# Attention scores as zero-padded single products between the matmuls of an MLP, instead of pairs on two halves of the TensorE array

## The reference

```python
# r, k, v: (B=4, H=8, S=768, D=48); w, u: (H, D)
for t in range(S):
    cur = einsum('bhd,bhe->bhde', u * k[t], v[t])
    y[t] = einsum('bhd,bhde->bhe', r[t], state + cur)
    state = w[..., None] * state + einsum('bhd,bhe->bhde', k[t], v[t])
x = y.transpose(0, 2, 1, 3).reshape(3072, 384)
h = x @ w_in;  x = (h * sigmoid(1.702 * h)) @ w_out      # d_ff = 2048
h = x @ w_in2; x = (h * tanh(softplus(h))) @ w_out2
```

## Time and profile before

| | us |
|---|---|
| median of 3 runs | 945.72 |
| lowest and highest | 943.12 and 946.43 |
| the profiled execution, its own time | 943.12 |
| its span in the trace | 941.0 |

### The profile page before, as it was taken

How to read it: one execution, slowest core, us unless ns; L and a number is a source line. 1 busy time by engine, 2 the same in 40 slices (tenths; PEclk the granted TensorE clock), 3 DMA queues, 4 the chain that set the end, 5 groups by cost and what they waited for, 6 DMA issues and landing times.

```text
span 941.0 us, 11881 instructions
## 1 busy us (share of the span) xinstructions
PE 929.4 (99%) x4716; PEld 777.1 (83%) x4716; DVE 397.7 (42%) x683; ACT 171.1 (18%) x314; POOL 183.0 (19%) x157
## 2 busy tenths in 40 slices
PE   8989999999999999999999999999999999999998
PEld 7878888888888888888888888888888888888886
DVE  8375663443454343444335543233233333233322
ACT  0322311111111111111123331111111111111111
POOL 6665743331323231333000000000000000000000
PEclk8599999999999999999999999999999999999999
DMA  9652111220212021111043000000000000000000
GB/s 213 156 177 68 43 34 51 55 51 22 59 50 52 26 67 44 34 51 42 1 151 92 27 1 1 1 34 0 1 34 1 34 1 1 33 1 1 34 1 33
DMA packets 41029, 41.85 MB, mean 44 GB/s; under 512 B 27280, under 2 KB 33552, under 8 KB 40976
## 3 DMA queue, kind: packets, MB, share of 16 engines
q1 hardware_dynamic: 40976, 41.10, 15.7%
HBM read 36.37 MB, written 4.72 MB: 44 GB/s over the span
## 4 chain that ended last, share of the span: by engine, by line
PE 98%; DMA 1%; issue 0%; SPq 0%; DVE 0%; ACT 0%
PE h L767 44%; PE acc L786 42%; PE y_bank L695 4%; PE a_bank L679 2%; PE y_bank L704 2%; PE z_bank L719 2%; PE z_bank L732 1%; DMA arena<-in_rk 1%; PE h L719 1%; PE acc L679 0%; PE y_bank L679 0%; DVE arena L510 0%; SPq L219 0%; DVE arena L487 0%; ACT arena L449 0%
## 5 line engine op out<-in xcount | busy, mean ns | idle before, releaser
L591 DVE CAST g_hi<-act 128x512 fp32r<-128x512 f32 x192 | 91.6, 477 | 410.9 <-PE acc L786 392.1
L427 ACT ACTIVATE act<-h 128x512 f32<-128x512 f32 x192 | 114.7, 597 | 547.8 <-PE h L767 547.8
L767 PE MATMUL h<-x_hi,win_hi 128*128 128x512 f32 x576 | 186.7, 407 | 0.7 <-ACT x_hi L413 0.7
L767 PE MATMUL h<-x_hi,win_lo 128*128 128x512 f32 x576 | 184.3, 409 | 0.0
L767 PE MATMUL h<-x_lo,win_hi 128*128 128x512 f32 x576 | 183.9, 409 | 0.0
L786 PE MATMUL acc<-g_hi,wout_hi 128*128 128x512 f32 x576 | 172.5, 399 | 0.0
L786 PE MATMUL acc<-g_hi,wout_lo 128*128 128x512 f32 x576 | 166.3, 390 | 0.0
L786 PE MATMUL acc<-g_lo,wout_hi 128*128 128x512 f32 x576 | 165.9, 389 | 0.0
L593 DVE TENSOR_TENSOR g_lo<-act,g_hi 128x512 fp32r<-128x512 f32 x192 | 146.9, 765 | 6.6
L786 PEld LDWEIGHTS acc<-g_hi,wout_hi 128*128 128x128 f32 x576 | 108.3, 188 | 23.7
L786 PEld LDWEIGHTS acc<-g_lo,wout_hi 128*128 128x128 f32 x576 | 108.1, 188 | 23.0
(11 more groups left out here) (102 smaller groups left out, 593.0 us busy)
## 6 DMA issues: line engine op xcount, KB each, us to landing
arena<-in_rk SPq DMA_DIRECT2D x44, 192.0 KB, 3.3
mid<-in_wts SPq DMA_DIRECT2D x16, 384.0 KB, 6.8
arena<-in_wts SPq DMA_DIRECT2D x16, 384.0 KB, 3.3
arena<-in_k SPq DMA_DIRECT2D x22, 192.0 KB, 3.2
arena<-in_v SPq DMA_DIRECT2D x22, 192.0 KB, 3.2
arena<-in_r SPq DMA_DIRECT2D x21, 192.0 KB, 2.9
out<-mid SPq DMA_DIRECT2D x5, 768.0 KB, 3.3
mid<-in_rk SPq DMA_DIRECT2D x4, 192.0 KB, 7.6
```

The source lines that it names most:

```text
L427: act.activation(act1[:, f % 2], h_bank[f % 2][:, :], GATES[layer]).then_inc(g_done, 1)
L591: dve.tensor_copy(g_hi[:, f % 2], act1[:, f % 2]).then_inc(ghi_done, 1)
L767: ins = pe.matmul(hb, w[:, f, kd, :], x[:, par, kd, :], start=i + kd == 0, stop=i == 2 and kd == KD - 1)
```

## The change

`kz` is a new buffer with the decayed k of both halves, each 112 partitions high: `kz[:, 0]` holds the even heads in partitions 0 to 47 and zeros elsewhere, `kz[:, 1]` the odd heads in 64 to 111 and zeros elsewhere. GpSimd clears it once and then, for each chunk, writes the two 48-partition parts, and scales r in a third operation. The score product of a half is then 112 rows deep, with the zeros taking out the other head. It stands alone after one MLP matmul, like the other pieces.

Both halves go through `a_bank` and one `amat` buffer, one after the other: half 0 in phase 0 (j = 0 to 3), half 1 in phase 1 (j = 4 to 7). `inside` of half 0 comes in phase 1 at j = 0 to 3, that of half 1 in phase 2 at j = 0 to 3, and `before` moves to j = 4 to 7 of phase 2. `y_bank` holds no scores any more, so the wait for `x_done` moves from `scores` to `inside`. `prepare` of a chunk waits until the scores of the chunk before have been computed (`a_done`), since there is one `kz`.

In the opening the products stay 48 rows deep and in their old banks, but all four of half 0 come first and then all four of half 1. The dummy matmuls become 20 of 128x128 in place of 8 of these and 24 smaller ones.

```diff
-WARM = 8
+WARM = 20
...
+        kz = part(2 * HP * CH)[0:PR_ROWS, :].rearrange("p (a h t) -> p a h t", a=2, h=HP)
...
-        amat = [part(HP * CH).rearrange("p (h t) -> p h t", h=HP) for _ in range(2)]
+        amat = part(HP * CH).rearrange("p (h t) -> p h t", h=HP)
...
+            pool.memset(kz, 0.0).then_inc(cleared, 1)
...
                 pool.wait_ge(rk_in[b], a * 32 + 32)
-                pool.tensor_tensor(e.rk, e.rk, decay, ALU.mult).then_inc(r_dec, 1)
+                pool.wait_ge(a_done, n * 2)
+                for j, p0 in enumerate((0, ODD)):
+                    if j:
+                        pool.wait_ge(kz_done, n * 2 - 2 * B + 1)
+                    pool.tensor_tensor(kz[p0:p0 + D, j], e.rk[p0:p0 + D, 1], decay[p0:p0 + D, 1], ALU.mult).then_inc(kz_done, 1)
+                pool.wait_ge(kz_done, n * 2 - 2 * B + 2)
+                pool.tensor_tensor(e.rk[:, 0], e.rk[:, 0], decay[:, 0], ALU.mult).then_inc(r_dec, 1)
...
-                if phase == 0 and b < B:
-                    for half in range(2):
-                        select(n, later[b], later_scores[half], half)
+                if phase < 2 and b < B:
+                    select(n, later[b], a_bank, phase)
...
+                else:
+                    if hp == 0:
+                        pe.wait_ge(kz_done, n * 2 - 2 * B + 2)
+                        pe.wait_ge(r_dec, n + 1)
+                        pe.wait_ge(sel_done, n * 2 + half)
+                    ins = pe.matmul(a_bank[:, hp * CH:(hp + 1) * CH], kz[:, half, hp, :], later[b].rk[:, 0, hp, :], start=True, stop=True)
...
-                    if phase == 0 and j == 0:
-                        scores(n, b)
-                    if phase == 1 and j // 4 < 2:
-                        inside(n, b, j // 4, i, a)
+                    if phase == 0 and j // 4 == 0:
+                        scores(n, b, 0, i)
+                    if phase == 1 and j // 4 == 0:
+                        inside(n, b, 0, i, a)
+                    if phase == 1 and j // 4 == 1:
+                        scores(n, b, 1, i)
                     if phase == 2 and j // 4 == 0:
+                        inside(n, b, 1, i, a)
+                    if phase == 2 and j // 4 == 1:
                         before(n, b, i)
```

More of the change, by code:

```diff
@@ L101, in operands @@
         def operands(b):
-            return Buffers(rk=rk[b % 2], ks=ks[b % 2], vs=vs[b % 2], rr=rr, amat=amat)
+            return Buffers(rk=rk[b % 2], ks=ks[b % 2], vs=vs[b % 2], rr=rr, amat=[amat, amat])
         STG0 = FIRST
@@ L147, in mlp_rwkv_program @@
         first_scores = [[a_bank, h_bank[0]], [acc[0], acc[1]]]
-        later_scores = [a_bank, y_bank]
         first_update = h_bank[1]
@@ L165, in mlp_rwkv_program @@
         dtab = sem("dtab")
+        kz_done = sem("kz_done")
         r_dec = sem("r_dec")
@@ L385, in chunk @@
                         split(f)
-            pool.wait_ge(cleared, 4)
+            pool.wait_ge(cleared, 5)
             pool.wait_ge(ds_done, B)
@@ L511, in _ @@
                 if b == 0:
-                    dve.tensor_tensor(amat[0][0:PR_ROWS], decay[:, 1], wide(powers[:, LOGS - 1, 0, :], CH), ALU.mult).then_inc(dsrc, 1)
+                    dve.tensor_tensor(amat[0:PR_ROWS], decay[:, 1], wide(powers[:, LOGS - 1, 0, :], CH), ALU.mult).then_inc(dsrc, 1)
             def split(win, wout):
@@ L665, in decay_rows, with scores @@
                 for hp in range(HP):
-                    ins = pe.transpose(z_bank[:, hp * PR_ROWS:(hp + 1) * PR_ROWS], amat[0][0:PR_ROWS, hp, :], ident[0:PR_ROWS, 0:PR_ROWS])
+                    ins = pe.transpose(z_bank[:, hp * PR_ROWS:(hp + 1) * PR_ROWS], amat[0:PR_ROWS, hp, :], ident[0:PR_ROWS, 0:PR_ROWS])
                 ins.then_inc(dtrn, 1)
[L669 to L682, removed]
+            def scores(n, b, half, hp):
+                if is_first(n):
+                    if hp == 0:
+                        pe.wait_ge(r_dec, n + 1)
+                        if n >= 2:
+                            pe.wait_ge(sel_done, (n - 2) * 2 + half + 1)
+                    p0, bank, r = ODD * half, first_scores[n % 2][half], first[b].rk
+                    ins = pe.matmul(bank[:, hp * CH:(hp + 1) * CH], r[p0:p0 + D, 1, hp, :], r[p0:p0 + D, 0, hp, :], start=True, stop=True)
+                else:
+                    if hp == 0:
+                        pe.wait_ge(kz_done, n * 2 - 2 * B + 2)
+                        pe.wait_ge(r_dec, n + 1)
+                        pe.wait_ge(sel_done, n * 2 + half)
+                    ins = pe.matmul(a_bank[:, hp * CH:(hp + 1) * CH], kz[:, half, hp, :], later[b].rk[:, 0, hp, :], start=True, stop=True)
+                if hp == HP - 1:
+                    ins.then_inc(a_done, 1)
             def inside(n, b, half, hp, a):
@@ L687, in inside @@
                 if hp == 0:
-                    pe.wait_ge(sel_done, n * 2 + half + 1 if is_first(n) else n * 2 + 2)
+                    pe.wait_ge(sel_done, n * 2 + half + 1)
                     if half == 0:
@@ L798, in _ @@
             pe.wait_ge(pattern, 4)
-            for i in range(WARM):
+            for _ in range(WARM):
                 pe.matmul(z_bank[:, 0:P], ident, mask, start=True, stop=True)
[L801 to L808, removed]
             for n in range(B + 2):
-                if n < B:
-                    scores(n, n)
+                for half in range(2):
+                    for hp in range(HP):
+                        if n < B:
+                            scores(n, n, half, hp)
                 if n == 0:
```

## The result

The changed kernel takes 955.75 us (median of 4 runs, 955.70 to 956.16) against 944.42 us for the kernel before (4 runs in all, 940.05 to 946.43): the ratio is 1.0128, with a 95% interval of 1.0089 to 1.0166. It is slower, by 11.3 us or 1.3%; +11.7 was forecast.

What follows compares the result with a forecast made beforehand. TensorE was taken to bound the kernel. Scores +10.4, waits -2.9 and opening +4.2 summed to +11.7 us, on the median of 945.7 giving 957.4 us; the forecast range 954.4 to 960 had 0.63.

Steps and rivals of the forecast that it cites:

- What bounds the kernel: Whole kernel: TensorE busy 929.4 of 941.0 us and 98% of the chain, so its program sets the time.
- Part 1: Scores beside the MLP, 20 chunks: single padded products cost 0.52 us more per chunk, +10.4 us (+10.2 to +11.0).
- the entry: Score block beside the MLP: getting in and out costs 0.44 us, which the change gets back.
- the price of a pass: Small products between MLP matmuls: 0.114 to 0.117 us a pass, set by weight load and not by columns.
- Part 2: Waits ahead of the scores in tile 0: they go as `inside` waits for `x_done`, -2.9 us (to -1.5).
- part 3: GpSimd's `prepare` as three operations, 3.8 us: hidden, 0 taken, up to 1 us at each of about three places.
- Part 4: DVE, SP and ACT: mask products and loads stay in time, 0, with 0.5 us at few places.
- Part 5: The opening: scores of chunks 1 to 3 lengthen as halves don't pair, +4.2 us (+2.3 to +5.2).
- the 16 passes one after the other: Opening scores: unpaired passes at 0.11 us, or 0.22 at low clock, adding 0.75 us (chunk 1), 1.7 (chunks 2, 3).
- A clock that rises sooner in the opening: Rival, opening: denser scores raise the clock sooner, saving 3 to 7 us, 950.4 to 954.4; chance 0.15.
- New waits: Rival, mainly tile 0: GpSimd's longer chain delays mask products or `win_ready`, +4 to +7 us, 961 to 964; chance 0.14.
- Cheap passes: Rival, scores beside the MLP: a padded pass costs half, 0.057 us, part 1 -8 us, total 939; chance 0.02.

Runs made afterwards that it cites:

- e6: The kernel before, with its four pairs of score products one after each of MLP matmuls j = 0 to 3 instead of in one block: 971.44 us.
- e4: The changed kernel with only 64 of 128 columns streamed in each score product beside the MLP, half of the scores left out: 953.54 us.
- e3: The changed kernel without zero padding: score products beside the MLP 48 rows deep, standing singly, k scaled in place: 1022.02 us.
- e2: The changed kernel with the four zero-padded products of a half in one block after one MLP matmul: 954.13 us.
- e1: The changed kernel, but in the opening the two halves of each score pair stand next to each other again: 952.78 us.
- e7: The changed kernel with the dummy matmuls of the kernel before: 956.04 us.
- e5: The kernel before, with its score block after matmul j = 8 of phase 0 instead of j = 0: 937.40 us against 943.31.

## Why the prediction was right, and where its steps were off

**What bounds the kernel: right.** TensorE's share of the chain is 98% before and after. GpSimd's busy time grew from 183.0 to 219.9 us and DVE's from 397.7 to 434.9, and TensorE waited less for its scores than before.

**Part 1, the scores: right in its mechanism, mis-sized by a fifth.** +0.52 us a chunk was forecast and 0.62 measured, 12.4 in place of 10.4 us over 20 chunks, beyond the stated bound of 11.0. That pairs are free and that columns don't count is shown by e6 and e4, the entry at 0.39 us by e3 and e6 (0.44 was read). The term that was mis-sized is the price of a pass, 0.122 us for 0.115. The missing 0.10 us is made of MLP matmuls that start 0.49 in place of 0.455 us before the next, three behind score products in each chunk and one behind `before` in every second, 3.5 x 0.03. Such a thing can't be seen in a trace in which 112-row products of 128 columns don't occur. e4 still has some of them and e2 loses most of the 0.10, so it is tied to products standing between MLP matmuls and not to their columns alone; what it is stays open. Of the price itself, the prediction's reason (the weight load and not the columns) is shown in its second half only.

**Part 2, the waits: right.** -2.9 with -1.5 as the other bound; -2.4 came out. What was named as late next, the mask product of half 0 behind other DVE operations, was in time in the changed kernel's trace and 1.1 us late in those of e1 and e7, where TensorE was sooner. The 0.3 us twice are GpSimd's scaling of r ahead of the scores of chunks 6 and 7, behind the low parts of the weights. That belongs to part 3, where slack of 1.45 us was found for `up` and the scores behind the same `prepare` were taken as far away. Three operations take 2 x 1.32 + 1.39 = 4.0 us on average, 3.8 was said. e5 shows that the waits didn't need the rest of the change: the block moved by itself takes out all of them.

**Part 4: right in the trace after, not in general.** No wait of TensorE for DVE beside the MLP is in its list, although DVE's operations grew longer with GpSimd busier (`g_lo`, L601, 0.89 us on average for 0.77). But e1 and e7, the same kernel beside the MLP, have one of 1.1 us, where up to 0.5 was allowed. So the 0 held in this trace probably because the low clock had delayed TensorE.

**Part 5, the opening: the right sum by two wrong terms.** +4.2 was forecast, +4.1 measured, and that the two agree is luck. The step that failed is the 16 passes one after the other: the last passes of half 0 and the first of half 1 run beside each other, as pairs on different rows of the array do in e6. On the timeline after, products into `a_bank` and into `h` alternate at 22.77 and 22.93. The scores of a chunk at the low clock cost 3.03 us, +1.0 and not +1.7, and in e4, whose opening had the high clock then, 1.64 for 1.10, +0.5 and not +0.75. That is 2.6 us for the order of the halves. Chunk 1 also started 0.3 us sooner. The other part is the clock, which in this execution fell 2.0 us sooner and made the scores of chunk 1 (3.02 for 1.64) and `inside` (3.45 for 3.00 us) 1.8 us slower. With the clock as in e3 or e4 the opening ends at 43.4 to 43.5 us. The prediction had the clock as a rival on the side of a gain only. Its sentence that the clock is back only once the MLP matmuls run holds for the trace before (46.0, after 41.8), not for e1 and e5 (41.3 before 42.3, 28.7 before 37.2).

**The rivals.** A clock that rises sooner in the opening, brought by denser scores: it didn't come in the changed kernel, whose clock in the trace fell sooner and came back later than before. It did come in the paired form, in e5. New waits: 0.6 us in the trace after and about 1.7 in e1 and e7, not 4 to 7. Cheap passes: excluded by the timeline after (0.122 us a pass) and by e4 and e2.

**The level.** The sum stood on the median, 945.7, and gave 957.4; with the median of all four runs, 944.4, it would have been 956.1, 0.4 above the measured 955.75. That is closer than the mechanism was priced. Between the two traces the terms add up to 14.4 us, not 11.7: 2.0 more for the scores, 0.5 less gained at the waits, 0.3 for the clock at the first MLP matmuls, 0.1 less for the opening. The medians differ by only 11.3, since the profiled execution before was a short one and the one after a long one. So the time was right in part by luck.

## What to carry to other kernels

Price a small matmul between large ones from a neighbour of the same kind, by the distance between starts: here each pass costs 0.11 to 0.12 us, whether it streams 48 or 128 columns. Two half-height products on different rows of the array cost one, but each run of them costs 0.4 us to enter and leave, so keep them paired and in one block; if they must be spread, fill the height with zeros. When a wait is what hurts, first move the waiting block within its program: one number, j = 8 for j = 0, took out all of the waits ahead of the scores at no cost, where the rebuilding paid 12 us for it. And ask of a wait that is absent from one trace whether it is absent only because something else was late there.

## What the runs showed of the hardware

- Changing between 48-row and 112- or 128-row products and back costs 0.39 us each time, whether one or two products stand between (e3, e6).
- 48-row products of different halves overlap even when written one half after the other: 16 passes took the time of about 14 (3.03 us at 0.22 us a pass).
- The same opening ended at 41.8 us in one execution and at 37.2 in another (the kernel before and e5), as the granted clock came back at 46.0 or at 28.7 us. The runs of the kernel before spread over 936 to 949 us; the five executions of the changed kernel took 955.7 to 957.3.
- The granted clock also fell to 0.50 beside the MLP, without an idle stretch of TensorE ahead of it: five times in e3, 17 us in all, where 48-row products stood singly between the MLP matmuls.
- A split of g on DVE took 3.18 us in e7, where its median is 0.43 us, while GpSimd went from one operation to the next.
